# Scores in three bursts of four doubles a group, and the keys' other half copied by DMA

## The reference

```python
scores = (1.0 / S) * np.matmul(z, z.transpose(0, 2, 1))      # z: 8 x 3072 x 64
x = u * np.matmul(np.maximum(scores, 0.0) ** 2, v)           # u, v: 8 x 3072 x 256
N, cap = 3072, N // E * 2                                    # E = 8 experts, cap = 768 rows each
expert = np.argmax(x @ w_gate, axis=1)                       # rows go to experts in order of token
h = np.maximum(np.einsum('ecd,edf->ecf', disp, w1), 0.0)     # disp: the kept rows of each expert
y = np.einsum('ecf,efd->ecd', h, w2)
out[i] = gate_w[i] * y[expert[i], pos[i]]                    # rows over the capacity are 0
```

## Time and profile before

| | before |
|---|---|
| median of 3 runs | 850.01 us (849.98 to 852.62) |
| profiled execution | 849.98 us, span 848.2 us |
| PE busy | 833.9 us (98%), 7714 matmuls |
| DVE busy | 631.1 us (74%) |
| ACT busy | 561.5 us (66%) |
| POOL busy | 167.4 us (20%) |
| chain that ended last | PE 92%, issue 4%, DVE 3% |

### The profile page before, as it was taken

One profiled execution on the slowest core, in us unless ns is written; L12 is line 12 of the kernel. 1 busy time (PEld: TensorE's weight loads), 2 busy tenths in 40 slices (PEclk: granted clock), 3 DMA queues, 4 the chain that ended last, 5 costly groups with the idle time before them and its releaser, 6 DMA issues.

```text
span 848.2 us, 24366 instructions
## 1 busy us (share of the span) xinstructions
PE 833.9 (98%) x7714; PEld 650.7 (77%) x7714; DVE 631.1 (74%) x1360; ACT 561.5 (66%) x873; POOL 167.4 (20%) x198
## 2 busy tenths in 40 slices
PE   6999999999999999999999999999999999999997
PEld 5777787778777777787787778777777777777776
DVE  7987877889899788887888988777465565556531
ACT  7977777778778779776778777677435424434422
POOL 2003202202311220220320320220211211211212
PEclk9999999999999999999999999999999999999999
DMA  7923353443423733323323334632616415414201
GB/s 286 403 80 113 105 170 121 124 145 133 149 55 118 281 94 120 124 65 113 119 65 121 130 94 152 245 74 62 172 45 156 153 39 155 155 45 147 56 19 37
DMA packets 108118, 106.90 MB, mean 126 GB/s; under 512 B 68397, under 2 KB 94202, under 8 KB 107072
## 3 DMA queue, kind: packets, MB, share of 16 engines
q1 hardware_dynamic: 99360, 85.71, 32.4%
q0 software_dynamic: 8736, 20.90, 6.9%
HBM read 40.03 MB, written 44.93 MB: 100 GB/s over the span
## 4 chain that ended last, share of the span: by engine, by line
PE 92%; issue 4%; DVE 3%; DVEq 1%; POOL 0%; SPq 0%; DMA 0%; ACT 0%; POOLq 0%; ACTq 0%
PE O L737 17%; PE O L739 16%; PE O L741 16%; PE Sc L862 15%; PE Sc L703 13%; PE O L885 3%; PE O L889 3%; PE O L887 3%; PE Sc L887 2%; PE Sc L889 2%; PE Sc L885 2%; DVE attn_hi L1019 1%; PE Sc L791 1%; DVE wparts L1284 0%; SPq L282 0%
## 5 line engine op out<-in xcount | busy, mean ns | idle before, releaser
L737 PE MATMUL O<-vS,attn_hi 128*128 128x256 f16 x1332 | 363.7, 273 | 1.4 <-DVE vS L1005 1.4
L741 PE MATMUL O<-vS,attn_lo 128*128 128x256 f16 x1332 | 363.0, 273 | 0.0
L739 PE MATMUL O<-vS,attn_hi 128*128 128x256 f16 x1332 | 363.0, 273 | 0.0
L499 ACT ACTIVATE attn<-Sc 128x768 f32<-128x768 f32 x225 | 172.7, 799 | 90.0 <-DVE attn_lo L1025 64.5
L1025 DVE TENSOR_TENSOR attn_lo<-attn,attn_hi 128x768 f16<-128x768 f32 x223 | 213.7, 958 | 7.7
L504 ACT ACTIVATE attn<-attn 128x768 f32<-128x768 f32 x225 | 185.2, 840 | 3.6 <-ACT xT L474 1.4
L737 PEld LDWEIGHTS O<-vS,attn_hi 128*128 128x128 f16 x1332 | 130.0, 98 | 39.2 <-issue 19.3
L1329 DVE SCALAR_TENSOR_TENSOR rawv<-Sc,rawv 128x768 f16<-128x768 f32 x63 | 60.1, 956 | 110.0 <-ACT rawv L622 60.7
L741 PEld LDWEIGHTS O<-vS,attn_lo 128*128 128x128 f16 x1332 | 130.2, 98 | 15.1
L739 PEld LDWEIGHTS O<-vS,attn_hi 128*128 128x128 f16 x1332 | 130.2, 98 | 13.9
L411 POOL DMA_INDIRECT disp<-xrow,slot x54 | 67.9, 1258 | 355.2 <-DVE slot L1201 344.2
(11 more groups left out here) (167 smaller groups left out, 1032.1 us busy)
## 6 DMA issues: line engine op xcount, KB each, us to landing
out<-empty SPq DMA_DIRECT2D x16, 1536.0 KB, 5.9
wraw<-in_moe_w SPq DMA_DIRECT2D x16, 1024.0 KB
rawv<-in_v SPq DMA_DIRECT2D x14, 768.0 KB, 7.6
ubuf<-in_u SPq DMA_DIRECT2D x19, 384.0 KB, 3.2
disp<-vS SPq DMA_DIRECT2D x8, 774.0 KB, 11.4
rawz<-in_z SPq DMA_DIRECT2D x3, 768.0 KB
q_now<-zP POOLq DMA_DIRECT2D x18, 96.0 KB, 2.0
q_now<-zQ POOLq DMA_DIRECT2D x18, 96.0 KB, 1.9
```

Source lines behind the costliest of these rows:

```text
L499: act.activation(attn[:, c % BUFS, :, :], Sp[:, score_banks(c), 0:GROUP], ACT.Relu).then_inc(s["relu_done"], 1)
L737: nc.tensor.matmul(o_part(t), hi, v[:, 0:D], start=c == 0 and j == 0 and t % 2 == 0, stop=False, skip_group_check=True)
L739: nc.tensor.matmul(o_part(t), hi, v[:, D:2 * D], start=False, stop=False, skip_group_check=True)
L741: ins = nc.tensor.matmul(o_part(t), lo, v[:, 0:D], start=False, stop=c == PAIRS - 1 and j == 1, skip_group_check=True)
```

## The change

`BURST` becomes 4: a burst makes four doubles and stands at c = 0, 4 and 8, in the peeled group at c = 2, 4 and 8, with `turn_over` behind the prelude's burst cut from 90 to 50. PSUM has room for three doubles of 384 columns; the fourth is made in three pieces of 128 columns a half, in the columns that the six banks have left (`score_place`). It comes first in the burst, and its readiness is told with that of the third. The burst waits once, for all relus of the burst before. The logits and counts move to the free columns of O's second bank; logits come behind the last tile of c = 3, counts behind the burst at c = 4. `END_AT` becomes 4. ACT's relus follow `RELUS`, its squares run four doubles ahead. The copy of the keys in the other half is made by DMAs from SP (`across`), one for the high and one for the low part of a slice: in the peeled group slice 2 ahead of the fills and slice 3 behind them, in groups with g > 3 behind the flag. Slices 0 and 1 are still copied by DVE. The values of `khi_ready` and `klo_ready` become eightfold. `k_next` holds only the four doubles' r-th chunks.

```diff
-BURST = 3
+BURST = 4
...
-        k_next = [sb(f"k_next{k}", [P, SLICE * P], F16) for k in range(2)]
+        k_next = [sb(f"k_next{k}", [P, BURST * P], F16) for k in range(2)]
...
-        Sp = ps("Sc", [P, 2 * BURST, 512], F32)
+        Sp = ps("Sc", [P, 2 * TILES, 512], F32)
...
-        def score_banks(c):
-            return slice(2 * (c % BURST), 2 * (c % BURST) + 2)
+        def score_place(c):
+            i = c % BURST
+            if i < BURST - 1:
+                return Sp[:, 2 * i:2 * i + 2, 0:GROUP]
+            return Sp[:, :, GROUP:GROUP + P].rearrange("p (t j) n -> p t j n", t=TILES)
+        def attn_place(c):
+            if c % BURST < BURST - 1:
+                return attn[:, c % BUFS, :, :]
+            return attn[:, c % BUFS, :, :].rearrange("p j (t n) -> p t j n", t=TILES)
...
-        small_logits = Sp[:, 0, 0:TILES * 2 * E]
-        small_counts = Sp[:, 0, COUNTS_FROM:COUNTS_FROM + (TILES + 1) * E]
+        small_logits = Oa[:, 1, D:D + TILES * 2 * E]
+        small_counts = Oa[:, 1, D + COUNTS_FROM:D + COUNTS_FROM + (TILES + 1) * E]
...
+            def across(to, h, made_parts):
+                own, out = half(h), half(1 - h)
+                for hi_or_lo, made, copied in ((0, "zhi_ready", "khi_ready"), (1, "zlo_ready", "klo_ready")):
+                    own16, to16 = ((zP, zQ), (zQ, zP))[(h + hi_or_lo) % 2]
+                    wait_apart(sp, s[made], made_parts)
+                    sp.dma_start(to16[out, bass.ds(to, SLICE * P)], own16[own, bass.ds(to, SLICE * P)]
+                                 ).then_inc(s[copied], 16)
...
+                    across(2 * SLICE * P, 1, 6)
...
+                    across(3 * SLICE * P, 1, 8)
...
+                def next_keys():
+                    to = ((n + 8) & 8) * (S // 8) + (g & 3) * (SLICE * P)
+                    with sp.If(g < 6):
+                        across(to, 0, (n & 120) + g * 2 + 2)
+                    with sp.Else():
+                        across(to, 1, (n & 120) + g * 2 + 2)
+                if not isinstance(n, int):
+                    only_if(sp, sp.snap(end) > 0, lambda: only_if(sp, g > 3, next_keys))
...
-                    wait_apart(pool, s[key], (m & 126) + 2)
...
+                for key in ("khi_ready", "klo_ready"):
+                    wait_apart(pool, s[key], (m & 120) * 8 + 32)
...
-                    pool.dma_start(k[:, :], z16[:, bass.ds((m & 8) * (S // 8), SLICE * P)]
-                                   ).then_inc(s["loaded_k_next"], 16)
+                    for r in range(2):
+                        chunks = z16[half(r), :].rearrange("p (c j n) -> p c j n", j=2, n=P)
+                        pool.dma_start(k[half(r), :].rearrange("p (c n) -> p c n", n=P),
+                                       chunks[:, bass.ds((m & 8) // 8 * PAIRS, BURST), r, :]
+                                       ).then_inc(s["loaded_k_next"], 16)
...
-                act.activation(attn[:, c % BUFS, :, :], Sp[:, score_banks(c), 0:GROUP], ACT.Relu
-                               ).then_inc(s["relu_done"], 1)
+                act.activation(attn_place(c), score_place(c), ACT.Relu).then_inc(s["relu_done"], 1)
...
+            do_relu(2, 2)
+            do_relu(3, 3)
+            do_square(2, 2)
+            v_hi(2 * UNIT, 2 * UNIT)
+            do_square(3, 3)
...
-                        if peeled:
-                            if c == 0 or c % BURST:
-                                do_relu(K0 + c + 2, c + 2)
-                            do_square(K0 + c + 2, c + 2)
-                            if c % BURST == 2:
-                                do_relu(K0 + c + 3, c + 3)
-                            if c == PAIRS - 1:
-                                do_square(K0 + c + 3, c + 3)
-                        elif c % BURST == 0:
-                            do_relu(K0 + c + 3, c + 3)
-                        elif c % BURST == 1:
-                            do_relu(K0 + c + 3, c + 3)
-                            do_relu(K0 + c + 4, c + 4)
+                        for k in RELUS[c % BURST]:
+                            do_relu(K0 + c + k, c + k)
+                        if not peeled and c == EXP_AT:
+                            act.wait_ge(s["below_ready"], n * 2)
+                            act.activation(ex[:, :, :], logit[:, :, :], ACT.Exp).then_inc(s["exp_ready"], 1)
...
-                        if not peeled:
-                            do_square(K0 + c + 3, c + 3)
+                        do_square(K0 + c + BURST, c + BURST)
...
-                            z_hi(3 * SLICE * P, 1, False, SLICE * P)
-                            z_hi(3 * SLICE * P, 1, True, SLICE * P)
-                        if peeled and c in V0_AT:
-                            v_hi(UNIT * (2 + V0_AT.index(c)), UNIT * (2 + V0_AT.index(c)))
...
+                            v_hi(UNIT * (3 + V0_AT.index(c)), UNIT * (3 + V0_AT.index(c)))
...
-                                    keys_high(ZHI_AT.index(c))
+                                    keys_high()
...
-                        wait_apart(pe, s[key], value)
...
-                        wait_apart(pe, s[key], value)
+                        wait_apart(pe, s[key], value * 8)
...
-                        pe.wait_ge(s[key], value)
+                        pe.wait_ge(s[key], value * 8)
...
-                if not isinstance(K, int):
-                    if par is None or c < PAIRS - BURST:
-                        wait_apart(pe, s["relu_done"], K - BURST + 1)
-                elif K >= BURST:
-                    pe.wait_ge(s["relu_done"], K - BURST + 1)
...
+                i = c % BURST
+                pieces = [slice(0, GROUP)] if i < BURST - 1 else [slice(t * P, (t + 1) * P) for t in range(TILES)]
...
-                    for r in range(2):
-                        ins = nc.tensor.matmul(Sp[:, 2 * (c % BURST) + r, 0:GROUP], keys[r], queries[r],
-                                               start=at == 0, stop=at == len(terms) - 1)
-                ins.then_inc(s["scores_ready"], 1)
+                    for t, columns in enumerate(pieces):
+                        for r in range(2):
+                            to = Sp[:, 2 * i + r, 0:GROUP] if i < BURST - 1 else Sp[:, 2 * t + r, GROUP:GROUP + P]
+                            ins = nc.tensor.matmul(to, keys[r], queries[r][:, columns],
+                                                   start=at == 0, stop=at == len(terms) - 1)
+                if i < BURST - 1:
+                    ins.then_inc(s["scores_ready"], 1 if i < BURST - 2 else 2)
+            def burst(K, n, c, par):
+                for k in (BURST - 1, *range(BURST - 1)):
+                    scores(K + k, n, c + k, par)
...
-            wait_keys(2, False)
-            for c in range(BURST):
-                scores(c, 0, c, 0)
-            turn_over(90)
+            wait_keys(4, False)
...
+                def counts_of_tiles():
+                    pe.wait_ge(s["onehot_ready"], n)
+                    counts = small_counts.rearrange("p (t e) -> p t e", t=TILES + 1)
+                    nc.tensor.matmul(small_counts, before[:, :], onehot[:, :, :].rearrange("p t e -> p (t e)"),
+                                     start=False, stop=False, skip_group_check=True)
+                    for k in range(TILES):
+                        ins = nc.tensor.matmul(counts[:, k + 1:TILES + 1, :], ones[:, :],
+                                               onehot[:, k:k + 1, :].to_broadcast([P, TILES - k, E]),
+                                               start=False, stop=k == TILES - 1, skip_group_check=True)
+                    ins.then_inc(s["counts_ready"], 1)
...
-                        def burst():
-                            first = c + BURST
-                            if first < PAIRS:
-                                if peeled:
-                                    wait_keys(2 * (first // BURST) + 2, False)
-                                for k in range(first, first + BURST):
-                                    scores(K0 + k, n, k, par)
-                            else:
-                                if not peeled:
-                                    wait_keys(((n + 1) & 120) + 6)
-                                for k in range(BURST):
-                                    scores(K0 + PAIRS + k, n + 1, k, 0 if peeled else None)
-                        if not peeled and c == 0:
+                        if peeled and c == FIRST_BURST_AT:
+                            wait_keys(6, False)
+                            pe.wait_ge(s["relu_done"], BURST)
+                            burst(BURST, 0, BURST, 0)
+                        elif c == 0 and not peeled:
...
-                        if not peeled and c == END_AT:
-                            wait_keys((n & 120) + 8)
-                            wait_apart(pe, s["relu_done"], K0 + PAIRS - BURST)
-                        if not peeled and c == PAIRS - BURST:
-                            wait_apart(pe, s["loaded_q_next"], n * 32)
```

(81 more changed lines are left out.)

55 lines of the change are left out of this document (20 added, 35 removed).

## The result

The changed kernel takes 869.67 us (median of 4 runs, 869.5 to 870.62), the kernel before beside it 850.15: ratio 1.0225, 95% interval 1.0205 to 1.0245. The profiled execution took 869.64 us, span 867.8. It is slower by 19.5 us; the forecast was slower by 8.9, 858.9 us with a range of 853.5 to 865.5. The direction was right, the size wrong.

A forecast was written before the change was run, and what follows sets the result against it. PE, busy 98% of the span, was taken to bound the kernel. Terms +8.3 + 2.1 - 3.4 + 1.3 - 1.0 - 0.5 + 3.1 - 1.0 = +8.9 on 849.98 gave 858.9 us, range 853.5 to 865.5.

The forecast's parts named there:

- fewer bursts and split double, groups 1 to 17: All groups: 18 fewer bursts, -3.4 us; the fourth double in nine 128-column pairs, 56 times on the path, +1.3 us.
- first group: start, wait at c = 1, pause: First group: weighing starts unchanged, +0.7 us idle before weigh 1, +7.6 waiting for slice 3's keys; +8.3 in sum.
- clock behind the pause: First group, after the pause: clock falls to half speed for about 4.2 us, +2.1 us, bounds 0 and 4.
- part 6: Logits: rows land 10.2 us after a group's end, PE is there at 10.14 and waits 0.2; +3.1 us in all.
- relus of a whole burst: Rival, chance 0.09: a whole burst's relus become a new wait, about 0.5 us at c = 4 in 17 groups; 867.
- rival of a clock that stays up: First group, chance 0.23: the clock does not fall over the pause; 856.8 us.
- unpaired pieces: Bursts, chance 0.08 with slow pieces: the fourth double's 128-column halves don't overlap; 886 us.
- slice in time: First group, chance 0.05: the fourth slice's last copy lands before 30.0 us, so no pause; 849.2 us.
- Part 3, the landing: First group: slice 3's last copy, queued behind the eighth fill, lands near 37.6 us; pause +7.6, bounds 6.5 and 9.
- Part 3, the start: First group: PE starts weighing at 19.25 us, unchanged.
- Part 5: Last group and end: one weighed double fewer, two more scored, -1.0 us; DVE's hi/lo pair gone, -0.5, bounds 0 and -1.
- Part 7: Two groups that reduce the norms: norms and the burst needing them stand a double sooner; -1.0 us, bounds -1.6 and +0.5.

The follow-up runs named there:

- e8: Changed kernel with slice 3's keys early and copied before the fills, rows' low parts sooner, flag behind double 5, first group's relu 7 sooner: 852.03 us.
- e1: Changed kernel with 156 products of 128 columns added in the first group ahead of PE's wait for keys at c = 4: 868.49 us.
- e6: Changed kernel with END_AT 5 instead of 4, so the flag is read behind double 5 as before the change: 867.37 us.
- e5: Changed kernel with six products of 128 columns added ahead of the logits' wait in every group but the first: 869.66 us.
- e10: Changed kernel with twelve products of 128 columns added ahead of the logits' wait: 880.86 us.
- e7: Changed kernel with DVE making the routed rows' low parts at c = 0 between do_hi(2) and do_lo(2), not behind both: 860.57 us.
- e2: Changed kernel with 90 instead of 40 warm-up products ahead of the first wait for keys: 871.72 us.
- e3: Changed kernel with SP sending the copies of keys' slice 3 before the eight fills of disp: 867.08 us.
- e9: Changed kernel with slice 3's other half in the first group written by ACT and DVE again instead of by DMA: 865.3 us.
- e4: Changed kernel with slice 3's high part made in the prelude, low part at c = 1, both copies sent before the fills: 860.24 us.

## Why the forecast was right in direction and wrong in size

The terms in the order of the forecast's sum:

| term | forecast | measured | from |
|---|---|---|---|
| fewer bursts and split double, groups 1 to 17 | -2.0 (17/18 of -3.4 + 1.3) | -3.1 | group without waits 30.50 (e8) for 30.68 |
| first group: start, wait at c = 1, pause | +8.3 | about +10.1 | +0.86, +0.44, +8.8 |
| clock behind the pause | +2.1 | +2.0 | e1 |
| leaving sooner, last group | -1.5 | -0.2 | marks above, e6 |
| logits wait | +3.1 | +2.6 | gaps ahead of L834, both kernels |
| behind the logits' wait | none | +5.0 | 17 x 0.29; e5, e10, e7 |
| reading the flag | none | +2.3 | gaps behind double 4; e6 |
| norms | -1.0 | +0.4 | gaps in the two groups |
| group 16, first burst | none | +0.7 | gap of 1.11 for 0.395 |

The measured column adds up to 19.8, and to 19.4 without the last group's own logits wait (0.4), which stands in it twice; the spans differ by 19.6.

**Right.** The pairs of 128 columns do pair: in the changed kernel's first burst at full speed they start at 24.65 and 24.70. The Trainium skill (TensorE: Matmul & The Clock Gate, Back-to-back issue gap) gives some 81 ns for a 128-column matmul with its weight load; here two of them, each on 64 rows of the array, take 55 ns together, so the trace disagrees, as the earlier trace rows did. The overhead of a burst is as before (0.205 and 0.255 at its ends). In part 6, rows that land 10.2 us after a group's end and PE there at 10.14 was right on both sides: they land at 10.2, and PE is there at 10.15 where nothing waits (e7). The relus of a whole burst cost nothing after the first group (group 1's first burst comes 0.23 us late, and the profile names no releaser). The clock did fall in the pause, so the rival of a clock that stays up is out; so are the unpaired pieces and the slice in time.

**Right in part by luck.** z_hi ran at 32.70 for a forecast 32.5, but PE's burst of c = 2 had started 0.6 us later than forecast (24.58 for 24.0). From that burst to z_hi pass 8.1 us, in e1 and e6 too (23.7 to 31.8), and the replay had 8.5; the late start made up for it. And the clock's price of 2.0 for 2.1 holds in this execution: from the burst of c = 4 to the end of the group the kernels in which the clock fell took 21.3 to 22.7 us against 19.87, a price of 1.4 to 2.8.

**Part 3, the landing.** The step that failed is "behind the two copies for slice 2 it moves by about 0.5". The eighth fill, which the copy queues behind, landed at 39.0 (26.4 + 12.6) instead of the forecast 36.8, and the low copy behind it at 39.44 instead of 37.6. The lines of the fills (L330), of the changed kernel and then of e1:

```profile
L330 SPq DMA_DIRECT2D disp<-vS x8: 444/1380/1795, 17.9 to 26.4; - x8
DMA to landing us min/median/max: 4.7/11.2/12.6
```

```profile
L330 SPq DMA_DIRECT2D disp<-vS x8: 433/1557/2333, 15.8 to 26.9; - x8
DMA to landing us min/median/max: 7.1/10.9/11.9
```

In the changed kernel the second copy took 2.61 us to issue and the fills began at 17.9 instead of 14.6. That is not what moved the landing: in e1 that issue took 0.51 us, the fills began at 15.8, and the eighth still landed at 38.8. In the kernels with the fills in this place it landed at 37.7 to 39.8, and the first fill already 1.0 to 3.0 us later than before. What holds the fills back behind two copies of 96 KB stays open. The step's upper bound, 9, held. e2 and e3 show the queue's share, e9 the whole way's.

**Part 3, the start.** "Unchanged" was wrong in this execution: the burst of four makes PE idle longer ahead of it, the clock fell, and ACT's first relu waited 1.1 us for the slow burst. I had weighed a fall for the long pause only. Of the ten kernels with 40 warm-up products the clock fell there in seven, and not in e1, e4 and e6. A second cause gives a late start too: in e4 it was 19.96 with the clock up, since the first piece of v landed at 7.8 instead of 6.85. With both well, in e1 and e6, it was 19.26 and 19.24, so this term is worth 0 to 0.9.

**Part 6, half priced.** The wait of 0.2 us was forecast and came, in the number of groups that was forecast. The failed step is that a wait costs its own length. In five of the groups before, logits waited and the next matmul still followed at 0.025: there a weighing came next. Now a burst with three waits of its own comes next, and after a wait that held nothing is queued to cover them. This alone is 5.0 of the 10.8 us that the forecast missed.

**Part 5, wrong sign.** "Bounds 0 and -1" took DVE's hi/lo pair to be what the end waits for, as it was before. In the changed kernel that pair is gone and DVE's last work ends at 610.76, but PE's product of `turn_over` starts only at 612.01, and the profile puts 0.68 us of idle time ahead of it down to DVE's queue (L1340, where DVE leaves its loop). What is left is the engines' leaving of their loops behind a flag that has only just come, and it is longer than the wait that went; and moving the read of the flag to the place where it is only just ready has a price in every group, for a gain that comes once.

**Part 7.** The wait at the burst went in the first of the two groups (0.6 us before) and stayed in the second (1.5 us, against 1.6). Their matmuls, now in the middle of a double, begin with a wait of their own (0.5 to 0.6 us in each).

The forecast's condition for being wrong was "groups 1 to 17 that differ from 30.7 by more than 0.3 us". They take 31.11, and its range had allowed nothing for a small loss in each of 17 groups except through a wait for relus.

## What to carry to other kernels

Ahead of a wait, ask not only how long it lasts but what stands behind it in the same engine's program: here PE's own waits and other instructions between logits and burst were free (0.10 us) as long as matmuls were queued ahead of them, and cost 0.39 behind a wait that held. A step that is moved to where its input is only just ready can cost a little in each turn (0.13 us here), so a gain that comes once must be set against it times the turns. And when the work of an engine is thinned, look at once for what may now be done sooner on it: here that was worth more than the thinning.

## What the runs showed of the hardware

- Behind a wait of PE that held, the next burst started 0.39 us after the last logits matmul, or up to 0.05 more, for waits of 0.1 to 0.7 us alike; 0.22 to 0.29 in most groups with 0.14 us of work left (e5), 0.10 with 0.47 (e10).
- The granted clock fell to 0.50 around 13 us in seven kernels, where PE had idled 2.7 to 3.9 us, in some of them only when the next matmuls had begun; in three with idle times of 3.1 to 3.4 us in the same place it stayed at 1.00 (e1, e4, e6). In e2 it fell 1 us into the work behind an idle time of 2.1 us. It stayed at 1.00 over 4.5 us at the end of the kernel before. The Trainium skill (TensorE: Matmul & The Clock Gate, What's actually happening) has the lower level as the default that activity lifts; e1, whose products kept the level at 1.00 through the same pause, agrees.
- The issue of a 96 KB copy on SP took 0.5 us at best and up to 2.61 in the changed kernel, with other DMAs in flight; in e1, in the same place, 0.51.
- In group 16, where the outer loop of PE's program turns, the burst at c = 0 starts 1.11 us behind the last weighing in the changed kernel (0.205 in most other groups), 0.89 to 1.11 in ten others, and 4.34 in e10. The profile names no releaser. In the kernel before the same burst starts 0.395 behind, the smallest of them. That it is the loading of the program's next piece is a guess; no run tested it.
